# Sixty-four weight columns in place of 128 in the low-half matmuls of a two-layer MLP's output rest

## What is computed

```python
def _moe_ref(x, w_in, w_out):
    h = np.maximum(x @ w_in, 0.0)
    return (h * h @ w_out).astype(np.float32)

def _moe2_ref(x, w_in, w_out):
    h = x @ w_in
    relu6 = np.clip(h + 3.0, 0.0, 6.0)
    g = h * relu6 / 6.0
    return (g @ w_out).astype(np.float32)

def reference(...):
    attn_out = _attn_ref(x, weight_gen)          # 2 x 4096 x 192
    x = attn_out.reshape(B * S, D)
    x = _moe_ref(x, w_in1, w_out1)               # w_in 192 x 2048, w_out 2048 x 192
    return _moe2_ref(x, w_in2, w_out2)
```

## Time and profile before

| | |
|---|---|
| median of 3 runs | 1126.94 us (1126.91 to 1126.97) |
| span of the profiled execution | 1125.2 us |
| PE busy in it | 1119.4 us (99%), 9940 matmuls |
| PEld busy in it | 1082.5 us (96%), 9940 loads |
| DVE, ACT busy | 906.8 us (81%), 668.8 us (59%) |
| granted TensorE clock | 9 in all 40 slices, that is 90% or more |

### The profile page before, as it was taken

One profiled execution on the slowest core, in us unless ns is written; L12 is line 12 of the kernel. 1 busy time (PEld: TensorE's weight loads), 2 busy tenths in 40 slices (PEclk: granted clock), 3 DMA queues, 4 the chain that ended last, 5 costly groups with the idle time before them and its releaser, 6 DMA issues.

```text
span 1125.2 us, 25509 instructions
## 1 busy us (share of the span) xinstructions
PE 1119.4 (99%) x9940; PEld 1082.5 (96%) x9940; DVE 906.8 (81%) x985; ACT 668.8 (59%) x747; POOL 3.1 (0%) x10
## 2 busy tenths in 40 slices
PE   9999999999999999999999999999999999999998
PEld 8998999999999999999999999999999999999997
DVE  8788796987969789697887978879698797976665
ACT  7986556565565655645556555555655556456554
POOL 1000000000000000000000000000000000000000
PEclk9999999999999999999999999999999999999999
DMA  7221002020110201103020020200202002010001
GB/s 214 86 66 36 6 16 63 4 74 7 30 48 3 75 6 57 25 0 77 4 66 15 0 77 4 70 11 8 69 4 73 8 17 59 0 40 4 1 16 29
DMA packets 79302, 41.28 MB, mean 37 GB/s; under 512 B 56172, under 2 KB 72300, under 8 KB 79272
## 3 DMA queue, kind: packets, MB, share of 16 engines
q1 hardware_dynamic: 79144, 40.64, 13.9%
q10 hardware_dynamic: 128, 0.22, 0.1%
HBM read 29.42 MB, written 11.40 MB: 36 GB/s over the span
## 4 chain that ended last, share of the span: by engine, by line
PE 99%; DVE 0%; DMA 0%; ACT 0%; issue 0%; DVEq 0%
PE h_ps L1131 46%; PE y_ps L1141 31%; PE y_ps L1149 21%; PE h_ps L988 0%; DMA wraw<-in_weight_gen_dram 0%; PE y_ps L1099 0%; PE y_ps L988 0%; PE y_ps L1272 0%; PE h_ps L1099 0%; PE y_ps L1253 0%; DVE prod L721 0%; PE y_ps L1254 0%; PE y_ps L1259 0%; PE y_ps L1256 0%; PE h_ps L1089 0%
## 5 line engine op out<-in xcount | busy, mean ns | idle before, releaser
L1131 PE MATMUL h_ps<-xt,win 64*128 64x512 f32 x4552 | 1026.4, 386 | 0.0
L1131 PEld LDWEIGHTS h_ps<-xt,win 64*128 64x128 f32 x4552 | 801.3, 184 | 14.9
L1141 PE MATMUL y_ps<-hid_hi,wout 64*128 64x512 f32 x2032 | 542.5, 386 | 0.0
L503 ACT ACTIVATE hid_hi<-hid 128x1024 fp32r<-128x1024 f32 x240 | 254.7, 1061 | 328.9 <-DVE hid L822 166.0
L831 DVE TENSOR_TENSOR hid_lo<-hid,hid_hi 128x1024 fp32r<-128x1024 f32 x253 | 309.5, 1223 | 147.6 <-ACT hid_hi L503 141.5
L1141 PEld LDWEIGHTS y_ps<-hid_hi,wout 64*128 64x128 f32 x2032 | 373.3, 184 | 7.1 <-PE y_ps L1141 0.3
L1141 PE MATMUL y_ps<-hid_lo,wout 64*128 64x512 f32 x1016 | 311.6, 386 | 0.0
L1149 PE MATMUL y_ps<-hid_hi,wout 64*128 64x512 f32 x1016 | 311.4, 386 | 0.0
L1149 PE MATMUL y_ps<-hid_lo,wout 64*128 64x512 f32 x1016 | 311.3, 386 | 0.0
L1141 PEld LDWEIGHTS y_ps<-hid_lo,wout 64*128 64x128 f32 x1016 | 186.8, 184 | 4.0 <-DVE hid_lo L806 0.3
L1149 PEld LDWEIGHTS y_ps<-hid_hi,wout 64*128 64x128 f32 x1016 | 186.9, 184 | 3.7 <-PE y_ps L1149 0.3
(11 more groups left out here) (116 smaller groups left out, 358.1 us busy)
## 6 DMA issues: line engine op xcount, KB each, us to landing
xwin<-in_x_dram SPq DMA_DIRECT2D x14, 960.0 KB, 5.9
by_feature<-stage SPq DMA_DIRECT2D x52, 96.0 KB, 2.0
out_dram<-outs SPq DMA_DIRECT2D x240, 16.0 KB, 1.5
out_dram<-outs SPq DMA_DIRECT2D x240, 8.0 KB, 1.4
stage<-by_feature SPq DMA_DIRECT2D x13, 256.0 KB, 3.0
stage<-in_moe_w_out_dram SPq DMA_DIRECT2D x8, 384.0 KB, 3.6
stage<-in_moe_w_in_dram SPq DMA_DIRECT2D x8, 256.0 KB, 3.7
stage<-in_moe_w_in_dram SPq DMA_DIRECT2D x16, 128.0 KB, 3.7
```

Source lines behind the costliest of these rows:

```text
L503: act.activation(hi, hid[:, slot], ACT.Copy).then_inc(hi_done, 1)
L1131: return pe.matmul(h_ps[:, s % 2, t, :], win[layer][r, wn, cols], src[r, xn, :], start=bool(rows) and n in (0, SHORT), stop=not rows and n ...
L1141: return pe.matmul(ps[:, 0, :], wout[layer][r, tile, w_cols], src, start=bool(rows) and s == 0 and n == 0, stop=not rows and s == STEPS - ...
```

## The change

The matmuls of the rest's outputs with the low halves of the inner activations take 64 weight columns, `HI_REST`, in place of the 128 of `HI_LO_REST`. They write partitions 0 to 63 of bank 1 and leave partitions 64 to 127 alone, which hold the sum with the low halves of the weights. So the product of low weight halves and low activation halves is no longer added. The number of matmuls, their order, their waits and their 512 moving columns are the same. `skip_group_check` is a note to the simulator and changes no instruction. Where `start` was `... and n == 0` it still is, and `stop` is still given with n == 3.

```diff
                 src = (hid_hi if n < 2 else hid_lo)[r, s % 2, t, :]
-                return pe.matmul(ps[:, 1, :], wout[layer][r, PAIR * s + t, HI_LO_REST], src,
-                                 start=bool(rows) and s == 0 and n == 0, stop=not rows and s == STEPS - 1 and n == 3,
-                                 tile_position=(r.start, 0))
+                w = wout[layer][r, PAIR * s + t, :]
+                if n < 2:
+                    return pe.matmul(ps[:, 1, :], w[:, HI_LO_REST], src, start=bool(rows) and s == 0 and n == 0, stop=False,
+                                     skip_group_check=True, tile_position=(r.start, 0))
+
+                return pe.matmul(ps[0:REST, 1, :], w[:, HI_REST], src, start=False, stop=not rows and s == STEPS - 1 and n == 3,
+                                 skip_group_check=True, tile_position=(r.start, 0))
...
-                main, rest = ps[:, 0, :], ps[:, 1, :]
+                main, rest, rest_high = ps[:, 0, :], ps[:, 1, :], ps[0:REST, 1, :]
...
                 for t, tile in enumerate(tiles):
-                    ins = pe.matmul(rest, w[:, tile, HI_LO_REST], los[:, t, :], start=False, stop=last and t == PAIR - 1)
+                    ins = pe.matmul(rest_high, w[:, tile, HI_REST], los[:, t, :], start=False, stop=last and t == PAIR - 1,
+                                    skip_group_check=True)
```

More of the change, by code:

```diff
@@ L1255, in output_sums @@
                 for t, tile in enumerate(tiles):
-                    pe.matmul(rest, w[:, tile, HI_LO_REST], his[:, t, :], start=False, stop=False)
+                    pe.matmul(rest, w[:, tile, HI_LO_REST], his[:, t, :], start=False, stop=False, skip_group_check=True)
                 pe.wait_ge(lo_done, g + 1)
                 for t, tile in enumerate(tiles):
-                    ins = pe.matmul(rest, w[:, tile, HI_LO_REST], los[:, t, :], start=False, stop=last and t == PAIR - 1)
+                    ins = pe.matmul(rest_high, w[:, tile, HI_REST], los[:, t, :], start=False, stop=last and t == PAIR - 1,
+                                    skip_group_check=True)
                 if last:
```

## The result

The changed kernel takes 1135.29 us (median of 4 runs, 1135.22 to 1135.34), the kernel before 1126.95 us beside it. The ratio is 1.0073, with a 95% interval from 1.0059 to 1.0087: slower by 0.7%. I had forecast 1126.9 us and a range from 1123.3 to 1128.5.

The account below looks back on a forecast made before the run. PE's pace was taken as the bound: span 1125.2 us plus 0 for loads, matmuls and outputs, plus 1.7 us between median and span, gave 1126.9 us. The range was 1123.3 to 1128.5 us, holding 0.87.

Parts of the forecast that it names:

- What bounds the kernel: Whole kernel: PE, busy 1119.4 of 1125.2 us, sets the time; only what changes PE's own pace can change it.
- The surcharge: Each half's matmul starts: 0.013 us beyond the 0.2133 us of 512 columns, belonging to each matmul, whatever its number of rows.
- The load's term, 0: Weight loads before narrow matmuls: hidden behind the half's previous matmul, so shortening them gains 0; other bound 28 us.
- the rival with exposed loads: All narrow matmuls' loads count after all: 28 us faster, 1099 us; chance 0.04, shared with the surcharge gone.
- the late load: At 24.83 us a load started 0.12 us late, yet the distance from the half's previous matmul stayed 0.23 us.
- The matmul's term, 0: Narrow matmuls on PE: same 512 moving columns, surcharge assumed unchanged, so 0 gained or lost.
- the bounds -6.8 and +1.5 us: Narrow matmuls, 512 times on the path: surcharge gone saves 6.8 us; 3 ns more each costs 1.5 us.
- a change of width empties the array: At switches between 128 and 64 weight columns: 0.2 us each, 406 or 203 us in all, 1533 or 1330 us; chance 0.05.
- that part of my argument: Narrow matmuls' built instructions: same group of all 128 array columns as wide ones, only 64 active, so the same layout.
- The surcharge following the columns: Narrow matmuls: surcharge halved, 1123.5 us, chance 0.15; gone, 1120.1 us, chance 0.04 shared with loads that count.
- The profile that I expected: Changed kernel's trace: low-half loads under 184 ns, starts 0.227 us apart, 886 matmuls in 100 us, PEld's share down, PE's unchanged.
- A small cost of a few ns for each narrow matmul: At each narrow matmul: a few ns, adding up to more than 2.25 us slower; chance 0.04.

Follow-up runs that it names:

- the bench: Separate kernel of matmul streams in the kernel's forms, computing nothing else and copying x to the output; all wide 226.67 ns, the change's pattern loses 33.3 ns a period.

## Why the prediction was wrong, point by point

- **What bounds the kernel: right.** PE's own beat sets the time; every loss above is a loss of beat, 254 times.
- **The surcharge belongs to each matmul and not to the halves' sharing: right.** One half alone and full-row matmuls keep 226.67 ns in the bench.
- **The load's term, 0: the wrong reading of the right row.** The cover is there: narrow loads gained nothing, and the 28 us of the rival with exposed loads were far off. But from the earlier trace rows I took only the distance right behind the late load, 0.227 us, and wrote that the load "could start 0.11 us later and cost nothing". The nine distances behind it lost 47 ns. A disturbance is paid later than where it stands.
- **The matmul's term, 0, with the bounds -6.8 and +1.5 us: the step that failed.** It measured +8.3 us. I weighed only what a narrow matmul takes itself. Measured, that is 9 ns in the one distance between two narrow ones, and the rest comes from wide matmuls behind them. The bound of 1.5 us was taken from the length of records (389 against 386 ns), which says nothing of distances: the narrow ones' records are 391 ns long on the mean, and the loss a step is 33.3 ns.
- **The rival "a change of width empties the array": wrong in mechanism and in size.** I had priced it at 203 or 406 us, by the 0.2 us of the one switch of rows. PEld stood idle for 0.9 us in all before the 1016 narrow loads, as the page shows above. The switch from 64 to 128 rows costs the same after the change, which the timeline shows at the end:

```profile
1123.04 0.62 PE L1154 MATMUL y_ps<-hid_lo,wout 64*64 64x512 f32 x2
1123.59 0.19 PEld L1257 LDWEIGHTS y_ps<-win,wout 128*128 128x128 f32 x1 [0.41 <-issue]
1123.59 0.50 PE L1257 MATMUL y_ps<-win,wout 128*128 128x512 f32 x1
```

  So the rule of the Trainium skill (TensorEngine Tiling (Array Packing), Key Properties), that changing the tiling mode drains the engine, fits the rows, where the one switch costs 0.2 us. It doesn't reach the change of width made here: no narrow matmul shows such a gap. Which column group the narrow instructions carry stands in no trace, so that part of my argument stays unshown.
- **The surcharge following the columns: wrong for 512 moving columns.** All-narrow streams are slower there. At 256 it is what one sees, 113.3 against 120.0 ns, which is 6.7 ns for half the columns. No row of the kernel before shows how 512 differs.
- **The load by the Trainium skill (TensorE: Matmul & The Clock Gate, LDWEIGHTS):** columns divided by 1.2 in ns would shorten it by 53 ns; the records shrank by 52 (184 to 132). The rule holds for the difference, while each record is 77 to 79 ns longer than the rule's figure, and it tells nothing of the kernel's time.
- **The profile that I expected: half right.** The loads did get shorter, but I had PEld's share going down by a few per cent, and it rose from 96% to 98%, with 879 matmuls in 100 us in place of 886.
- **"A small cost of a few ns for each narrow matmul", 0.04:** the nearest of my cases, though 33.3 ns for two is 17 ns each and most of it isn't paid there. The share was too small for what I knew: no row held two widths side by side, so the only bounds that I had were from uniform streams.

## What to carry to other kernels

When a matmul stream is the bound and runs in an even beat, don't count an edit of one matmul by that matmul: read the distances between starts for ten matmuls behind the nearest irregularity in the old trace, such as a late load or a stall, and add up what they lose. Less work in one of them (fewer weight columns, fewer moving columns) can make the stream slower or give only a quarter of what it should. If narrow ones are needed, where they stand counts: with one wide matmul between two of them they cost 20 ns, side by side 33, far apart 40; and if two halves of the array wait for each other, the slower half's loss is the whole loss.

## What the runs showed of the hardware that I had not expected

- Fewer weight columns can be slower: matmuls of 512 moving columns in fp32r start 226.7 ns apart with 128 columns, 230.0 with 96 and with 64, and 231.7 with 32. With 256 moving columns it is the other way, 120.0 ns with 128 and 113.3 with 64.
- After most disturbances a stream takes 3 to 10 distances to return to its beat (one of 496 moving columns took none), in a chain of distances whose members are the same to 1 or 2 ns in the kernel before, the kernel after and the bench, with one half of the array, with both or with all rows.
- A loss in one half of the array is not added to the other's: with narrow matmuls in the upper half alone the kernel takes 1135.17 us, with them in both 1135.29 us.
